# One more fold of a two-dimensional Fourier transform on TensorE, and a new order of the stages around it

## The reference

```python
# 1 attention: a pooled one (mean over 4 tokens, repeated) plus a band of |i - j| < 4
out_d = sm_attn(q_d, k_d, v_d)
out_up = np.repeat(out_d, factor, axis=2)
attn_out = out_up + out_local
# 2 mixing and a wide layer (512 -> 2048 -> 512)
X = np.fft.fft(x, axis=1)
X = np.fft.fft(X, axis=2)
u = x + np.real(X)
un = (u - mu) / np.sqrt(var + 1e-06)
x = u + np.maximum(un @ w_ch1, 0.0) @ w_ch2
# 3 gated convolution (512 -> 1024 -> 512)
h = np.maximum(x @ w_in, 0.0)
out = (h * sigmoid(conv3(h))) @ w_out
```

## Time and profile before

| | |
|---|---|
| median of 3 runs | 845.96 us (844.97 to 846.36) |
| the profiled execution | 844.43 us, span 842.6 us |
| mean granted TensorE clock | 0.998 |
| PE busy | 823.0 us (98% of the span) |
| DVE, ACT, POOL busy | 431.3, 301.7, 263.4 us |
| DMA | 49.64 MB in 79490 packets, 60225 of them under 512 B |

### The profile page before, as it was taken

One profiled execution on the slowest core, in us unless ns is written; L12 is line 12 of the kernel. 1 busy time (PEld: TensorE's weight loads), 2 busy tenths in 40 slices (PEclk: granted clock), 3 DMA queues, 4 the chain that ended last, 5 costly groups with the idle time before them and its releaser, 6 DMA issues.

```text
span 842.6 us, 15876 instructions
## 1 busy us (share of the span) xinstructions
PE 823.0 (98%) x6420; PEld 739.4 (88%) x6420; DVE 431.3 (51%) x812; ACT 301.7 (36%) x879; POOL 263.4 (31%) x342
## 2 busy tenths in 40 slices
PE   8998999999999999999999999999999999999998
PEld 8677799998999899999998788888889889898986
DVE  5766745556443434564753131222227867477563
ACT  4664553446133341332322222212124343335332
POOL 2896774268220555160000405051510500000000
PEclk9999999999999999999999999999999999999999
DMA  9952432134101103300033101010100010010101
GB/s 210 250 125 72 100 75 59 40 88 114 45 15 41 56 17 125 101 26 26 26 129 129 63 0 63 1 62 1 63 1 1 1 51 1 9 55 1 51 1 62
DMA packets 79490, 49.64 MB, mean 59 GB/s; under 512 B 60225, under 2 KB 69209, under 8 KB 79418
## 3 DMA queue, kind: packets, MB, share of 16 engines
q1 hardware_dynamic: 77706, 44.37, 19.3%
q10 hardware_dynamic: 1712, 4.26, 1.4%
HBM read 39.18 MB, written 9.45 MB: 58 GB/s over the span
## 4 chain that ended last, share of the span: by engine, by line
PE 89%; DVE 4%; POOL 2%; DMA 2%; ACT 1%; issue 1%; SPq 1%; DVEq 0%
PE banks L806 14%; PE banks L823 13%; PE banks L941 12%; PE banks L958 11%; PE banks L915 10%; PE banks L900 10%; PE banks L764 4%; PE banks L737 3%; PE banks L711 2%; PE banks L640 2%; PE banks L626 2%; PE banks L673 1%; PE banks L659 1%; POOL w1aL L1635 1%; PE banks L685 1%; PE banks L696 1%
## 5 line engine op out<-in xcount | busy, mean ns | idle before, releaser
L806 PE MATMUL banks<-unH,w1aH 128*128 128x256 f32 x288 | 85.0, 295 | 0.4 <-DVE hL L1332 0.4
L823 PE MATMUL banks<-hH,w2aH 128*128 128x256 f32 x288 | 84.4, 293 | 0.0
L1464 DVE SCALAR_TENSOR_TENSOR hw<-banks,hw 128x512 fp32r<-128x512 f32 x32 | 22.1, 691 | 120.3 <-ACT hw L1125 120.3
L1673 POOL TENSOR_TENSOR accw<-accw,rstd_bc 128x512 f32<-128x512 f32 (+1 forms) x20 | 23.7, 1216 | 191.6 <-DVE accw L1348 88.4
L823 PE MATMUL banks<-hL,w2aH 128*128 128x256 f32 x288 | 81.4, 283 | 0.0
L806 PE MATMUL banks<-unL,w1aH 128*128 128x256 f32 x288 | 81.4, 283 | 0.0
L806 PE MATMUL banks<-unH,w1aL 128*128 128x256 f32 x288 | 81.4, 282 | 0.0
L823 PE MATMUL banks<-hH,w2aL 128*128 128x256 f32 x288 | 81.3, 282 | 0.0
L900 PE MATMUL banks<-unw,w1bH 128*128 128x512 f32 x256 | 78.9, 389 | 1.0 <-DVE unw L1459 1.0
L915 PE MATMUL banks<-hw,w2bH 128*128 128x512 f32 x256 | 79.0, 390 | 0.8 <-DVE hw L1464 0.8
L1056 ACT ACTIVATE hH<-banks 128x256 fp32r<-128x256 f32 x80 | 30.7, 383 | 134.5 <-PE banks L806 134.5
(11 more groups left out here) (192 smaller groups left out, 2157.7 us busy)
## 6 DMA issues: line engine op xcount, KB each, us to landing
qk_in<-in_q SPq DMA_DIRECT2D x32, 144.0 KB, 2.8
qk_in<-in_k SPq DMA_DIRECT2D x32, 144.0 KB, 2.9
v_grp<-in_v SPq DMA_DIRECT2D x16, 288.0 KB
acc_dram<-astage SPq DMA_DIRECT2D x9, 512.0 KB, 2.6
accw<-acc_dram SPq DMA_DIRECT2D x9, 512.0 KB, 4.8
out<-ostage SPq DMA_DIRECT2D x16, 256.0 KB, 2.7
v_win<-in_v SPq DMA_DIRECT2D x32, 122.5 KB
w2araw<-in_moe_w_ch SPq DMA_DIRECT2D x4, 512.0 KB, 7.5
```

The source lines that it names most:

```text
L806: last = nc.tensor.matmul(bank[0][:, 0:CT], w[wp][:, t, P * m:P * m + P], (unH, unL)[xp][:, t, :], start=(t == 0 and i == 0), stop=(t == P ...
L823: last = nc.tensor.matmul(bank[1 + d // 2][:, CT * (d % 2):CT * (d % 2) + CT], w[wp][:, m, P * d:P * d + P], (hH, hL)[xp][:, m % 2, :], st ...
```

## The change

1. **One more fold in both directions.** `fold` makes quarter sums and differences of the even half (`quart_p`, `quart_v`) and folds these again; it then writes six pieces where it wrote four. The three row groups of a transform become 128, 89 (87 for sines) and 72 rows. `fold_q` on DVE folds the feature tiles once more. A feature unit is now two matmuls of 128 columns, one of 65 or 64 and one of 64; a sequence unit is two of 144, one of 73 and one of 72. They write every second or every fourth column of PSUM, so `keep_cos` and `keep_sin` copy straight.
2. **Cosines ahead of sines**: the three cosine units of a batch come first, and `fold`, `fold_d` and `fold_q` are cut by kind, so that cosine units need cosine pieces alone.
3. **A new `PLAN`** of 1329 stages; `warm` stages are 11 with 38 matmuls.
4. **Three places.** The load of `accw` goes out ahead of SP's wait for `rstd_kept`, and `flip_rstd` stands two stages earlier. POOL's last `finish` no longer waits for the fourth `hgL` and then runs in one piece: each of its eight operations waits for one more step of the second batch. The last stored tile is copied and stored in two halves, the second from ACT's queue.

```diff
 def transform_feat(b, r, kind):
-                unit = 2 * r + kind
-                for par in range(2):
-                    for j in range(2):
-                        last = nc.tensor.matmul(dft_bank(b, unit)[0:count, 129 * par:129 * par + n],
-                                                (plus, xs)[par][:, j, cols], trigd[:, j, par, kind, 0:n],
-                                                start=(j == 0), stop=(j == 1))
+                unit = 3 * kind + r
+                if kind:
+                    pe.wait_ge(cos_kept, 3 * b + r + 1)
+                if r == 0:
+                    pe.wait_ge(g_p, 4 * b + 2 * kind + 2)
+                    pe.wait_ge(g_v, 4 * b + 2 * kind + 2)
...
+                for j in range(2):
+                    first = 258 + odds * (2 * j + kind)
+                    nc.tensor.matmul(at[:, 1:256:2], xs[:, j, cols], trigd[:, first:first + odds], start=(j == 0), stop=False)
+                if r == 0:
+                    pe.wait_ge(g_q, 4 * b + 2 * kind + 2)
+                nc.tensor.matmul(at[:, 0:4 * fours:4], xs[:, 2, cols], trigd[:, 65 * kind:65 * kind + fours],
+                                 start=False, stop=False)
+                nc.tensor.matmul(at[:, 2:256:4], xs[:, 3, cols], trigd[:, 130 + twos * kind:130 + twos * kind + twos],
+                                 start=False, stop=True).then_inc(s1_full, 1)
 def transform_seq(b, i, kind):
-                for r, dst, start, n in ((1, slice(0, NK), 0, NK), (0, slice(0, NK, 2), NK, HS // 2 + 1),
-                                         (2, slice(1, NK, 2), NK + HS // 2 + 1, HS // 2)):
+                for r, n_rows, dst, start, n in ((1, ROWS[kind][1][1], slice(1, NK, 2), 0, Q4),
+                                                 (0, ROWS[kind][0][1], slice(1, NK, 2), Q4, Q4),
+                                                 (0, FOURTHS[kind], slice(0, NK, 4), 2 * Q4, TWOS + 1),
+                                                 (2, TWOS, slice(2, NK, 4), 2 * Q4 + TWOS + 1, TWOS)):
 def fold_q(b, kind):
+                nc.vector.tensor_tensor(xs[:, 2, cols], plus[:, 0, cols], plus[:, 1, cols], ALU.add).then_inc(g_q, 1)
+                nc.vector.tensor_tensor(xs[:, 3, cols], plus[:, 0, cols], plus[:, 1, cols], ALU.subtract).then_inc(g_q, 1)
 PLAN
-    flip_q.2 centre_w1.0.0 load_q.3 round_w2.0.1 norm_l.1.1 centre_w1.0.1 norm_d.1 round_w1.0.0 low_w2.0.1 warm.7
+    join.2.1 top_l.4.0 norm_d.3 flip_p.3.1 keep_p0.3 score_d.4 keep_p1.3 fold.2 centre_w1.0.2 exp_l.4.0 flip_pd.3
...
 def store_rstd():
+                sp.wait_ge(a_stored, 16 * NCH)
+                sp.wait_ge(var_full, B)
+                sp.dma_start(accw[:, :, 0:CT], acc_d[0]).then_inc(b_loaded, 16)
                 sp.wait_ge(rstd_kept, 1)
 def finish(ch, cols, to):
+                    if ch == NW:
+                        pool.wait_ge(hgL_ok, M2 + d)
...
+                    if ch == NW:
+                        pool.wait_ge(hgL_ok, M2 + PB + d)
 def batch(b, last_one):
+                        parts = column_halves if last_one and tt == FULL - 1 else (slice(0, D),)
```

More of the change, by code:

```diff
@@ L26, in feature_table @@
 def feature_table(D):
[L28 to L32, removed]
-def fold_rows(S):
-    q = S // 4
-    cos = [(s, 0, 0.5 if s == q else 1.0) for s in range(q + 1)] + [(s, 1, 1.0) for s in range(q)]
-    sin = [(s, 0, 1.0) for s in range(1, q)] + [(s, 1, 0.5 if s == q else 1.0) for s in range(1, q + 1)]
+    p = np.arange(P)[:, None]
@@ new lines @@
+    contract.0.2 join.7.0 keep_q.9 weigh.7.1 fold.6 expand.0.4 join.7.1 low_w2.0.3 contract.0.3 relu.0.4 mask.8.1
+    exp_l.8.0 split.0.4 fold.7 expand.0.5 fold_d.1.0 contract.0.4 relu.0.5 split.0.5 invert.8.0 expand.0.6 top_l.8.1
+    fold_s.1 contract.0.5 norm_l.8.0 relu.0.6 split.0.6 fold_d.1.1 expand.0.7 round_u.1.0 fold_q.1.0 fold_d.1.2
+    flip_k.9 relu.0.7 exp_l.8.1 feat.1.0.0 fold_q.1.1 load_k.10 feat.1.1.0 low_u.1.0 load_q.10 keep_cos.1.0 feat.1.2.0
+    keep_cos.1.1 feat.1.0.1 keep_cos.1.2 invert.8.1 turn.1.0 feat.1.1.1 keep_sin.1.0 keep_k.9 feat.1.2.1 keep_sin.1.1
@@ new lines @@
+    keep_pd.11 mask.12.1 contract.2.0 relu.2.1 exp_l.12.0 split.2.1 fold.10 load_vg.12 top_l.12.1 pooled.11
+    store_acc.1 flip_q.13 keep_up.11 weigh.11.0 expand.2.2 join.11.0 contract.2.1 relu.2.2 fold_d.2.0 split.2.2
+    expand.2.3 weigh.11.1 relu.2.3 exp_l.12.1 contract.2.2 join.11.1 split.2.3 fold.11 expand.2.4 contract.2.3
+    fold_d.2.1 relu.2.4 split.2.4 fold_q.2.0 expand.2.5 fold_s.2 invert.12.0 contract.2.4 relu.2.5 fold_d.2.2
+    keep_q.13 invert.12.1 pool_q.13 fold_q.2.1 feat.2.0.0 feat.2.1.0 keep_cos.2.0 feat.2.2.0 split.2.5 keep_cos.2.1
@@ new lines @@
+    exp_l.15.1 split.4.2 invert.15.0 expand.4.3 norm_l.15.0 invert.15.1 pooled.14 relu.4.3 norm_l.15.1 flip_p.15.0
+    keep_up.14 norm_d.15 flip_p.15.1 weigh.14.0 fold.13 contract.4.2 join.14.0 keep_p0.15 split.4.3 weigh.14.1
+    expand.4.4 join.14.1 keep_p1.15 flip_pd.15 relu.4.4 fold.14 split.4.4 contract.4.3 keep_pd.15 pooled.15 expand.4.5
+    keep_up.15 fold_d.3.0 weigh.15.0 relu.4.5 split.4.5 contract.4.4 join.15.0 weigh.15.1 expand.4.6 join.15.1 fold.15
+    load_w1.1.0 load_w1.1.1 contract.4.5 relu.4.6 load_w1.1.2 store_acc.3 split.4.6 load_w1.1.3 fold_s.3 expand.4.7
@@ L205 @@
+    contract.9.5 relu.9.6 load_wi split.9.6 low_w2.1.3 flip_rstd expand.9.7 keep_rstd store_rstd contract.9.6 relu.9.7
+    split.9.7 contract.9.7
 """.split())]
@@ L1271, in fold_d @@
[L1271 to L1277 removed]
+                for u, op in enumerate((ALU.add, ALU.subtract)):
+                    nc.vector.tensor_tensor(half_v[:, u, 0:HS], x[:, 0:HS], x[:, HS:S], op).then_inc(halved_v, 1)
```

438 lines of the change are left out of this document (231 added, 207 removed).

## The result

The changed kernel takes a median of 823.73 us (823.12 to 824.7, four runs) against 846.16 for the kernel before: a ratio of 0.974 (95% interval 0.971 to 0.977). The forecast was 822 in a range of 812 to 833. The profiled execution took 823.74 us, 20.7 less than before's 844.43; the sum of steps said 24.0 less.

A forecast was written before the change was run, and what follows sets the result against it. PE, busy 98% of the span, was taken as the bound. 844.43 - 2.5 - 1.6 - 13.4 - 1.9 - 1.8 - 2.6 - 0.2 = 820.4 us profiled; plus 1.5 for the median gave 822, range 812 to 833.

The forecast's parts named there:

- the sum of steps: Whole kernel: all terms taken from the profiled execution's 844.43 us, giving 820.4 us.
- The price of a record: Transform matmuls: each record costs the longer of weight load and moving columns, plus 3 ns; features -2.5 us, sequence units -1.6.
- columns rule: Rival on transform matmuls: loads hide deeper than one record, so columns alone count; 8.8 us less, 813; chance 0.10.
- The start: Stretch before the first transform matmul: it starts at 63.0 instead of 74.46 us; with 2.0 us of work done earlier, -13.4 us.
- the transfers set the start: Rival on the start: the full SP queue is the pace; of 13.4 us some 3 stay, 832; chance 0.12.
- The half clock: First transform's feature records: PE expected at 2.4 GHz where part ran at 1.2 GHz; -1.9 us, otherwise 0.
- New waits in the mixed stretch: Rival: folds and fold_q stand between split stages on DVE; ten waits of 0.5 us, 827; chance 0.12.
- Costed at nothing: DVE's extra work, about 3 us a batch, hidden by PE's expand and contract stages; POOL's extra folds likewise; 0 us.
- From the transform to the wide pass: First transform matmul to last narrow contract: transforms -4.1, half clock -1.9, work done earlier 1.9; together -7.9 us.
- Wide pass: Start of the wide pass: both PE waits for DVE, 1.03 and 0.75 us, go; -1.8 us.
- `finish`: Last layer's first batch: POOL's work moves to the second batch, whose slack covers it; 50.49 to 47.85, -2.6 us.
- The last store: End of the span: half a tile is shorter to move; -0.2 us, between +0.2 and -0.5.

The follow-up runs named there:

- both experiments: Changed kernel plus a start block of compute-nothing matmuls in eleven shapes: 111 ns with 128 weight, 16 moving columns; changed kernel, 73-column sequence matmuls widened to 128: 823.54 us.
- POOL's queue alone: Kernel before with its four low_w1 stages (sixteen POOL operations) moved behind the first transform, all 79 warm matmuls kept: 846.81 us.
- the warm matmuls alone: Kernel before with its warm matmuls cut from 79 to 38 and nothing else: 847.35 us.
- the order of the transfers: Changed kernel with seven first-layer weight loads again ahead of the q and k loads of units 2 and 3: 835.72 us, ratio 0.989.
- the late loads: Kernel before with first-layer weight loads and the work on them at the change's places: 867.24 us with 79 warm matmuls, 867.55 with 38.
- the run of single records: Changed kernel plus a start block of 30 compute-nothing float32 matmuls for each of eleven weight and moving widths; 111 ns a record at 128 weight, 16 moving columns.

## Why the prediction was right, and where it was not

The range and the sign held, and the forecast lay 1.7 us below the median. That it lay so near is in part luck. The sum gave 820.4 for the profiled execution, which took 823.74: 3.3 us short. The forecast then added 1.5 us, since before's median lay that far above its profiled execution; here the two are equal. Before's runs spread with their mean clock (841.49 us at 0.999, 850.3 at 0.992, in one group of seven), the changed kernel's hardly do (823.12 to 824.7). Point by point:

- **The price of a record**: right, and shown by both experiments. Features -2.5 forecast, 4 x (5.26 - 4.62) = -2.6 measured; sequence units -1.6 forecast, -1.7 measured. The rival "columns rule" is out: weights of 128 columns cost 111 ns with 16 moving columns as with 128. By the Trainium skill's page "TensorE: Matmul & The Clock Gate", section "LDWEIGHTS (loading the stationary operand)", 128, 96, 72 and 64 weight columns take 107, 80, 60 and 53 ns (an estimate from its formula). The distances of this case, 111, 80 (scaled from 160 at 1.2 GHz), 64 and 58, agree within 5 ns.
- **The start**: the size nearly, the cause wrong. The step that failed is "I take 63, since POOL's queue is what the warm matmuls were bridging". POOL's queue alone moved nothing and the warm matmuls alone gained nothing, while the order of the transfers was worth 12.0 us in the changed kernel. It is needed and not enough: in the old order of units the late loads came with a slower kernel. The rival "the transfers set the start" had the right limit and the wrong sign: it took the change to leave the limit in place, while the change's new order of loads is what relieves it. I had the row for this (SP's queue at 104%) and read it as a brake on the gain. The gain came out 3.1 us short. The 2.69 us stall at 62 us is most of it, and the half clock behind it adds to it (twelve records of L678 took 1.71 us there, 0.90 at full clock). `fold_d` on POOL did end early, at 56.5 us (forecast 58.9).
- **The half clock** of -1.9: gone from the transform, but not from the kernel. Batch 0's feature records took 4.93 us (7.14 before). Before lost 1.7 us to the half clock behind its wait at 74 us (0.21 of 8 us); the changed kernel loses 1.8 us between 56 and 72 us (0.06 and 0.16 of 8) and 1.7 at 121 to 129. It comes behind stalls, and these moved; at the start it comes in some executions and not in others, so that a term for it is no better than a mean.
- **New waits in the mixed stretch** (rival, 0.12): the one that counts came at one place instead of ten, but with 2.60 us instead of 0.5, since I took the duration of a DVE operation alone, "PE stands for one DVE operation, 0.50 us". The operation was a wide one beside a busy POOL, 4.39 us.
- **Costed at nothing** failed at the same two places, and by one mechanism: DVE's and POOL's extra folds are hidden on average (54% and 34% busy), not where both run at once.
- **From the transform to the wide pass** 7.5 us went, of 7.9 forecast, although a new stall stood against it. In the chains the feature records took 18.8 us instead of 23.1 and the sequence units 30.1 instead of 31.8, and 1.9 us of work had been done earlier: 8.0 together. PE's idle time there (length less busy time of the window) is 3.4 us before and 3.7 after, and the half clock at 121 to 129 us costs 1.7. That would leave 6.0; where the other 1.5 us went I did not resolve.
- **Wide pass**: its two waits (1.78 us) are gone, as forecast. Of the other 0.6 us, 0.25 are the transpose of `flip_rstd` (L849), which stood behind the last narrow contract and now stands ahead of it, no gain; most of the rest went with the second wait, behind which twelve records took 3.01 us where twelve take 2.72.
- **`finish`** -2.6: right. **The last store** -0.2: wrong sign. The second half tile is copied by the same DVE after the first, and the span ends 4.2 us behind PE instead of 4.0, at the upper end of its bounds.

## What to carry to other kernels

A float32 matmul costs the longer of its weight load and its moving columns: a fold pays where it makes the weight tile narrower or leaves matmuls out, and by its moving columns only as long as these are no fewer than the weight columns. An engine that is busy all of a window is not therefore what the others wait for; take its work away in thought and ask what is late next, and give a full DMA queue that place first. Of an operation on DVE or POOL take the duration beside the other engine, not alone, and lay it where the other rests. Before you credit an edit with a clock of 1.00, look at the same stretch in runs that leave it alone.

## What the runs showed of the hardware

**DVE and POOL keep each other out for longer than one operation.** One DVE operation with two SBUF inputs takes 1.22 us beside an idle POOL and 4.39 beside a busy one. POOL's q_pool takes 0.45 us alone and 2.60 while DVE runs seven folds in a row, from 57.77 to 59.5 us. Two of them, in DVE's timeline:

```profile
57.77 0.81 DVE L1289 TENSOR_TENSOR half_v<-xT 128x288 f32<-128x288 f32 x2
```

The Trainium skill's page "SBUF — State Buffer", section "SBUF: two separate sides", says that of a DVE operation with two SBUF inputs and a POOL operation that reads SBUF, whichever starts first has the shared ports for its whole instruction and the other is blocked. The traces agree that the loss depends on the other engine being busy, but not with the bound that this gives. The 2.15 us that q_pool lost are more than any one DVE operation beside it (0.69 us at most). The 3.2 us that the DVE operation lost are more than any one POOL operation beside it (1.31 us at most). So the loser misses more than one turn. The starts and ends of POOL's operations are rough in a trace, but the delays are also seen in PE's stalls of 2.69 and 2.60 us.

**The clock can fall while PE never stops.** In the run of single records PE was busy 2.00 of every 2 us, yet the granted clock went from 1.00 to 0.50 (1.2 GHz) among the records with 16 moving columns, stayed there through those of 96 weight columns, and came back at 56.3 us, where the last of these meet the first of 72 weight and 128 moving columns; it fell again at 73.4 us, at the records with 17 moving columns:

```profile
36.00:38.00 2.00, 2.00 (x21) 2.00 (x19) 0.00 (x0) 0.00 (x0) 0.00 (x0) 1.00 0.00 0
38.00:40.00 2.00, 2.00 (x17) 2.00 (x17) 0.00 (x0) 0.00 (x0) 0.00 (x0) 0.82 0.00 0
40.00:48.00 8.00, 8.00 (x41) 8.00 (x41) 0.00 (x0) 0.00 (x0) 0.00 (x0) 0.50 0.01 2
```

I had expected the clock to go only with a wait of PE; none of these windows has one.
